# Banded attention and two MoE layers in one program: a shorter routing chain with narrow products, and a new order at both ends of attention

## The reference

```
x   = attention(q, k, v)      # 4 batches, 8 heads, 768 positions, 64 wide
      # own window of |i-j| < 16, and 24 block summaries of 32 keys each
      # (max of keys, mean of values), one softmax over both
y   = moe1(x)                 # 3072 tokens x 512, 8 experts of 512-1024-512
      logits = x @ w_gate
      for (token, expert) by falling logit:    # greedy, one assignment a token
          take it if the token is free and the expert has < 384 tokens
      out[token] = relu(x @ w1[e]) @ w2[e]
out = moe2(y)                 # tokens with y @ w_skip > 0: top-1 expert,
                              # y + gate * ffn(y); others are copied
```

## Time and profile before

| | |
|---|---|
| median of 3 runs | 844.89 us |
| the profiled execution | 845.31 us, span 843.5 us |
| PE matmul busy | 797.3 us (95%) |
| VectorE busy | 465.2 us (55%) |
| ScalarE, GpSimd busy | 228.2 and 216.0 us |
| granted clock, mean | 0.992 |

### The profile page before, as it was taken

How to read it: one execution, slowest core, us unless ns; L and a number is a source line. 1 busy time by engine, 2 the same in 40 slices (tenths; PEclk the granted TensorE clock), 3 DMA queues, 4 the chain that set the end, 5 groups by cost and what they waited for, 6 DMA issues and landing times.

```text
span 843.5 us, 15049 instructions
## 1 busy us (share of the span) xinstructions
PE 797.3 (95%) x4960; PEld 510.3 (61%) x4960; DVE 465.2 (55%) x2146; ACT 228.2 (27%) x681; POOL 216.0 (26%) x313
## 2 busy tenths in 40 slices
PE   5999997797899999999999999999999999999996
PEld 5878785786345445454554545555577686777762
DVE  6989895677777676776767677607049100000000
ACT  5878785421102121121211212121111111110101
POOL 6888973001021020302102021120300321211110
PEclk9999999899999999999999999999999999999999
DMA  9976650436071440706225071446987999898983
GB/s 260 279 235 208 222 151 2 181 129 224 6 262 51 142 170 3 283 26 222 90 75 211 26 261 51 148 164 240 361 321 293 414 372 348 308 338 310 332 318 105
DMA packets 64506, 171.66 MB, mean 204 GB/s; under 512 B 5585, under 2 KB 5585, under 8 KB 64449
## 3 DMA queue, kind: packets, MB, share of 16 engines
q1 hardware_dynamic: 54512, 143.70, 48.3%
q0 software_dynamic: 6480, 20.91, 6.8%
q10 hardware_dynamic: 3456, 6.29, 1.9%
HBM read 148.41 MB, written 22.81 MB: 203 GB/s over the span
## 4 chain that ended last, share of the span: by engine, by line
PE 75%; DVE 14%; DMA 4%; issue 3%; POOL 3%; ACT 1%; DVEq 0%; SPq 0%; POOLq 0%; ACTq 0%
PE bank L1433 16%; PE bank L1447 16%; PE bank L1575 11%; PE bank L1557 11%; DVE junk L987 4%; PE bank L1301 4%; PE bank L1328 3%; PE bank L1310 3%; PE bank L1506 2%; DMA weights<-in_moe_w 1%; PE bank L1298 1%; PE bank L1422 1%; PE bank L1633 1%; PE bank L1601 1%; PE bank L1646 1%
## 5 line engine op out<-in xcount | busy, mean ns | idle before, releaser
L1433 PE MATMUL bank<-features,weights 128*128 128x384 f32 x512 | 182.3, 497 | 0.6 <-ACT features L749 0.6
L1447 PE MATMUL bank<-weights 128*128 128x512 f32 x384 | 179.2, 602 | 0.0
L987 DVE TENSOR_SCALAR_CACHE_REDUCE junk<-Vt,cand 128x192 bf16<-128x192 f32 x376 | 136.1, 410 | 4.8
L1433 PEld LDWEIGHTS bank<-features,weights 128*128 128x128 f32 x512 | 89.5, 191 | 50.6 <-issue 5.6
L1557 PEld LDWEIGHTS bank<-x2T,weights 128*128 128x128 f32 x896 | 102.2, 192 | 5.9 <-issue 5.9
L1557 PE MATMUL bank<-x2T,weights 128*128 128x128 f32 x896 | 102.6, 275 | 0.0
L1447 PEld LDWEIGHTS bank<-weights 128*128 128x128 f32 x384 | 66.8, 190 | 58.5 <-issue 56.5
L1575 PE MATMUL bank<-weights,h2T 128*128 128x512 f32 x224 | 98.8, 593 | 0.4 <-ACT h2T L816 0.4
L1147 DVE SCALAR_TENSOR_TENSOR o<-bank,gate,x 128x512 f32<-128x512 f32 x14 | 10.5, 751 | 154.5 <-PE bank L1575 154.4
L754 ACT ACTIVATE weights<-bank 128x384 f32<-128x384 f32 x64 | 31.4, 490 | 141.4 <-PE bank L1433 141.4
L1575 PEld LDWEIGHTS bank<-weights,h2T 128*128 128x128 f32 x224 | 41.3, 190 | 46.5 <-issue 46.5
(11 more groups left out here) (324 smaller groups left out, 1048.3 us busy)
## 6 DMA issues: line engine op xcount, KB each, us to landing
weights<-in_moe_w SPq DMA_DIRECT2D x52, 2048.0 KB, 9.6
vw<-in_vwin SPq DMA_DIRECT2D x16, 576.0 KB, 4.9
qc<-in_qT SPq DMA_DIRECT2D x16, 384.0 KB, 5.3
kc<-in_kT SPq DMA_DIRECT2D x16, 384.0 KB, 5.8
vc<-in_vT SPq DMA_DIRECT2D x16, 384.0 KB, 7.4
x_rows<-xr SPq DMA_DIRECT2D x24, 256.0 KB, 2.2
y_rows<-weights ACTq DMA_DIRECT2D x24, 256.0 KB
weights<-x_rows,gidx POOLq DMA_INDIRECT x24
```

The lines of the kernel that those rows point to most:

```text
L987: ins = ve.tensor_scalar(junk[:, c, :], Vt[:, :], cand[:, c:c + 1].bitcast(fp32), 0.0, ALU.is_ge, ALU.add, accum_out=cnt[:, c:c + 1])
L1433: ins = mm(HB[r % 2][:, 0:CAP], w1[:, c, 128 * r:128 * r + 128], xgT[:, c, :], start=(c == 0), stop=(c == KC - 1))
L1447: ins = mm(YB[j % 2][:, :], hT[:, r, 128 * j:128 * j + 128], w2[:, r, :], start=(r == 0), stop=(r == FC - 1))
```

## The change

- Narrow products: CNT, TAU, BAS go to 8, 8 and 2 columns; BASN is accumulated into BAS through shifted columns of `rowt`.
- VectorE's chain after the rounds: two operations on oneE are fused into others, the ranks are prepared while PE makes the base, and the expert's number is sent after the row totals, not before; oneE itself is made after the slots. For the first list of tokens, fold and ids are taken some operations earlier.
- End of attention: the first maximum and V are made in two parts, 18 tiles during groups 42 to 45, the last 6 tiles after the last logits. PE transposes six tiles of x before the rounds, and has fillers there.
- Start of attention: SP loads a pair's value windows after the next pair's queries and keys; VectorE takes pair 1's block maxima earlier and its key windows before the first reciprocal; PE has seven products that nothing reads while it waits for the first scores.
- The three gathered columns have a semaphore each; window 1 allows its work one round earlier, 161 units for 145.

```
-        VTP, CNT, TAU = SM[:, 0:256], SM[:, 256:256 + WIDE], SM[:, 384:384 + WIDE]
+        VTP, CNT, TAU = SM[:, 0:256], SM[:, 256:264], SM[:, 384:384 + E]
-            for u in range(NB):
+            load_qk(0)
+            load_columns(0)
+            for u in range(1, NB):
                 load_qk(u)
+                load_v(u - 1)
                 load_columns(u)
-                load_v(u)
+            load_v(NB - 1)
...
+            block_maxima(0)
             first_windows(0, NG)
             block_sums(0)
             maxima(0)
+            block_maxima(1)
             maxima(1)
+            first_windows(1, 1)
             recip(0)
-            first_windows(1, 1)
             maxima(2)
             block_sums(1)
...
+            known, final = slice(0, NT - TB), slice(NT - TB, NT)
...
+                if n == NG * (U - 2):
+                    dve.wait_ge(s["logit_in"], B - 1)
+                    best_of(known)
+                if n == NG * (U - 2) + 1:
+                    dve.wait_ge(s["rev_ready"], 1)
+                    first_of(known)
+                if n == NG * (U - 2) + 2:
+                    others_out(known)
+                if n == NG * (U - 2) + 3:
+                    open_values(known)
             logits_in(B - 1)
             dve.wait_ge(s["logit_in"], B)
+            best_of(final)
+            first_of(final)
+            others_out(final)
+            open_values(final)
...
                 o.step(ve.tensor_reduce(m, src, X, ALU.max))
+                if first_list:
+                    fold_out(ids_of)
                 o.step(ve.tensor_tensor(tmp, src, bc(m, shape, 2), ALU.is_equal))
-                if ids_of is not None:
+                if first_list:
+                    ids_out(ids_of)
+                elif ids_of is not None:
                     fold_out(ids_of)
...
-                o.step(ve.tensor_scalar(oneE[:, :], TAU[:, 0:E], tau[:, :], None, ALU.is_equal))
-                o.step(ve.tensor_tensor(oneE[:, :], oneE[:, :], revE[:, :], ALU.mult))
+                o.step(ve.scalar_tensor_tensor(out=oneE[:, :], in0=TAU, scalar=tau[:, :], in1=revE[:, :],
+                                               op0=ALU.is_equal, op1=ALU.mult))
                 o.step(ve.tensor_reduce(oneM[:, :], oneE[:, :], X, ALU.max))
-                o.step(ve.tensor_scalar(oneE[:, :], oneE[:, :], oneM[:, :], None, ALU.is_equal))
+                o.step(ve.scalar_tensor_tensor(out=t1[:, :, :], in0=bc(oneE[:, :], full, 1), scalar=oneM[:, :], in1=V[:, :, :],
+                                               op0=ALU.is_equal, op1=ALU.mult))
+                o.step(ve.tensor_reduce(mx[:, :], t1[:, :, :], X, ALU.add))
...
+                ve.tensor_copy(rowt[:, 1:3], scn[:, :, NT - 1]).then_inc(s["rows_ready"], 1)
+                o.step(ve.scalar_tensor_tensor(out=rank[:, :, :], in0=scn[:, :, :], scalar=float(-BIG_SLOT), in1=GT[:, :, :],
+                                               op0=ALU.add, op1=ALU.subtract))
                 o.step(ve.tensor_scalar(e_f[:, :], oneM[:, :], -1.0, float(E), ALU.mult, ALU.add))
...
                 ve.tensor_copy(e_i[:, :], e_f[:, :]).then_inc(s["expert_ready"], 1)
+                dve.wait_ge(s["base_mm"], ph + 1)
                 for h in range(2):
+                    o.step(ve.scalar_tensor_tensor(out=rank[:, h, :], in0=rank[:, h, :], scalar=BAS[:, h:h + 1],
                                                    in1=GT[:, h, :], op0=ALU.add, op1=ALU.mult))
...
                 o.step(ve.tensor_scalar(sel[:, :], slot[:, :], CAP - 0.5, None, ALU.is_lt))
+                o.step(ve.tensor_scalar(oneE[:, :], oneE[:, :], oneM[:, :], None, ALU.is_equal))
...
+            pe.wait_ge(s["pads_ready"], 1)
+            for _ in range(7):
+                mm(LG[0:32, 0:128], wg2[:, 0, :], wg2[:, :, :].rearrange("p c e -> p (c e)"), start=True, stop=True)
             pe.wait_ge(s["zeros_ready"], NB)
...
             logit_rows(B - 1)
+            for t in range(4):
+                x_rows_tile(t)
...
-                    return [0] + [0, 0, 6] + [6] * (ROUNDS - 3) + [15, 28, 4, 8]
+                    return [0] + [0, 6] + [9, 6, 6] * 5 + [16, 22, 4, 8]
...
-                if j == 0:
-                    pe.wait_ge(s["xg_in"], 16 * CT * (k + 1))
+                pe.wait_ge(s[f"xg_in{j}"], 16 * (k + 1))
...
+                keep_busy(w, 3)
                 pe.wait_ge(s["v_ready"], w + 1)
...
+                if w == 0:
+                    x_rows_tile(4)
+                    x_rows_tile(5)
+                keep_busy(w, 2)
                 for n in range(ROUNDS):
                     pe.wait_ge(s["cnt_ready"], ROUNDS * w + n + 1)
-                    mm(CNT, same_e[:, :], cnt[:, :].unsqueeze(1).to_broadcast([128, WIDE // 8, 8]),
-                       start=True, stop=True).then_inc(s["cnt_mm"], 1)
+                    mm(CNT, same_e[:, :], cnt[:, :], start=True, stop=True).then_inc(s["cnt_mm"], 1)
...
-                mm(BAS, tri[:, :], rowt[:, :], start=True, stop=True)
-                mm(BASN, ones_bf[:, :], rowt[:, :], start=True, stop=True).then_inc(s["base_mm"], 1)
+                mm(BAS, tri[:, :], rowt[:, 1:3], start=True, stop=False)
+                mm(BAS, ones_bf[:, :], rowt[:, 0:2], start=False, stop=True).then_inc(s["base_mm"], 1)
```

More of the change, by code:

```diff
@@ L106, in banded_attention_two_moe_layers @@
         steps3 = sb("steps3", [128, 3, 3], i32)
-        diag = sb("diag", [E, WIDE])
+        diag = sb("diag", [E, E])
         tau = sb("tau", [128, 1])
@@ L114, in banded_attention_two_moe_layers @@
         scn = sb("scn", [128, 2, NT])
-        rowt = sb("rowt", [128, WIDE], bf16)
-        base = sb("base", [128, 4])
+        rowt = sb("rowt", [128, 3], bf16)
+        rank = sb("rank", [128, 2, NT])
         slot = sb("slot", [128, NT])
@@ L380, in load_weights @@
                 if rows_first:
-                    sp.wait_ge(s["xg_in"], 16 * CT)
+                    for j in range(CT):
+                        sp.wait_ge(s[f"xg_in{j}"], 16)
                 sp.dma_start(W2[:, 2 * par, :].rearrange("p (c f) -> p c f", c=FC),
@@ L608, in _ @@
             keep_ids(0)
-            pool.wait_ge(s["xg_in"], 16 * CT)
+            for j in range(CT):
+                pool.wait_ge(s[f"xg_in{j}"], 16)
             with pool.Fori(1, E) as ph:
@@ L615, in _ @@
                 keep_ids(ph)
-                wait(pool, "xg_in", 16 * CT * (ph + 1))
+                for j in range(CT):
+                    wait(pool, f"xg_in{j}", 16 * (ph + 1))
                 o.leave(E)
@@ L908, in evac_pT, with bc, part_of, best_of @@
                 ve.tensor_copy(pT[:, n % 2, :], PT[n % 2][0:KW, :]).then_inc(s["prob_evac"], 1)
+            def bc(ap, shape, axis):
+                return ap.unsqueeze(axis).to_broadcast(shape)
+            known, final = slice(0, NT - TB), slice(NT - TB, NT)
+            def part_of(ts):
+                return [128, ts.stop - ts.start, E]
+            def best_of(ts):
+                o.step(ve.tensor_reduce(mx[:, ts], LM[:, ts, :], X, ALU.max))
+                o.step(ve.tensor_tensor(t1[:, ts, :], LM[:, ts, :], bc(mx[:, ts], part_of(ts), 2), ALU.is_equal))
+            def first_of(ts):
+                o.step(ve.tensor_tensor(t1[:, ts, :], t1[:, ts, :], bc(revE[:, :], part_of(ts), 1), ALU.mult))
+                o.step(ve.tensor_reduce(first[:, ts], t1[:, ts, :], X, ALU.max))
+            def others_out(ts):
+                o.step(ve.tensor_tensor(t1[:, ts, :], t1[:, ts, :], bc(first[:, ts], part_of(ts), 2), ALU.is_equal))
+                o.step(ve.tensor_scalar(t1[:, ts, :], t1[:, ts, :], -NEG, NEG, ALU.mult, ALU.add))
+            def open_values(ts):
+                o.step(ve.tensor_tensor(V[:, ts, :], LM[:, ts, :], t1[:, ts, :], ALU.add))
             def logits_in(b):
@@ L955, in first_max @@
                 o.step(ve.tensor_tensor(is_first, tmp, bc(first[:, 0:count], shape, 2), ALU.is_equal))
-                if ids_of is not None:
+                if ids_of is not None and not first_list:
                     ids_out(ids_of)
@@ L1010, in search @@
                                                        op0=ALU.logical_shift_left, op1=ALU.bitwise_xor))
-                ve.tensor_scalar(diag[:, 0:E], ident[0:E, 0:E], cand[0:E, 0:1].bitcast(fp32), None, ALU.mult) \
+                ve.tensor_scalar(diag[:, :], ident[0:E, 0:E], cand[0:E, 0:1].bitcast(fp32), None, ALU.mult) \
                     .then_inc(s["tau_diag"], 1)
                 dve.wait_ge(s["tau_mm"], ph + 1)
-                o.step(ve.tensor_reduce(tau[:, :], TAU[:, 0:E], X, ALU.max))
-                o.step(ve.tensor_scalar(oneE[:, :], TAU[:, 0:E], tau[:, :], None, ALU.is_equal))
-                o.step(ve.tensor_tensor(oneE[:, :], oneE[:, :], revE[:, :], ALU.mult))
+                o.step(ve.tensor_reduce(tau[:, :], TAU, X, ALU.max))
+                o.step(ve.scalar_tensor_tensor(out=oneE[:, :], in0=TAU, scalar=tau[:, :], in1=revE[:, :],
```

(4 more changed lines are left out.)

49 lines of the change are left out of this document (23 added, 26 removed).

## The result

The changed kernel takes **854.5 us** (median of 4 runs, 852.81 to 856.17) against 845.15 us for the kernel before beside it (844.82 to 845.77): ratio 1.0096, 95% interval 1.0068 to 1.0124, so it is slower by 1%. (The ratios here are the ones on record with their intervals; they differ by up to 0.0016 from the quotient of the two medians.) Forecast were 831.4 us and a range of 827 to 837, and faster. The profiled execution took 852.81 us with a span of 851.0.

The account below looks back on a forecast made before the run. PE work was taken as the main bound (75% of the span, VectorE 14%). V(2) earlier -5.3, lead -3.45, windows 2 to 7 -4.8: -13.5 from 845.31 gave 831.8, adjusted to the median 831.4 us; range 827 to 837.

Parts of the forecast that it names:

- the lead: Window 1: PE does 161 units for 145, so four second-layer products no longer follow, -3.45 us.
- rival D: Six full windows: PE, being ahead, waits for late gathered columns, up to 3.54 us each; 853 us, chance 0.04.
- The expert's number: After tau: number and weight load come 1.8 us later; weights landed long before use in window 0, so no charge.
- Narrow products in the full windows: Windows 2 to 7: each 8-column count product saves 0.03 us of PE's chain, 3.1 us in all.
- Rival B: Full windows: narrow products cost what wide ones did, next weights uncovered; 3.1 + 1.0 go, 835.5 us, chance 0.09.
- Windows 2 to 7 as a sum: PE-bound windows: count products 3.1, tau and base 1.0, shorter VectorE chain 0.7; -4.8 us, bounds 1 and 7.
- Start: Start of attention: keys loaded earlier and PE at full clock bring the fourth scores forward, -1.8 us, bounds 0.8 and 2.6.
- the signs: Start of attention: fourth scores near 12.8, first scores in about 1.05 us, V's first transpose near 147.5.
- Window 0: First window: head -0.9, rounds -1.0 and the search's tail -0.8 us.
- The store of tile 1: Head of window 0: if it again takes 4.58 us to land, round 1 goes only at 154.5, no gain.
- the forecast 191: Tail of window 0: sign that gidx, for the first list of tokens, would be done near 191.
- rival A: The ends give little: interleaved transfers, late store, gather and fillers taking 1.5 in window 1; 834.8 us, chance 0.18.

Follow-up runs that it names:

- e1_early: The changed kernel with the expert's number sent early again, as before the change, lead of 16 units kept: 848.19 us, ratio 1.002.
- e3_both: The changed kernel with the expert's number early and the old window 1 list (145 units, no lead): 837.84 us, ratio 0.9891.
- e7_lead17: The changed kernel with the expert's number early and one more unit in window 1's list (162 for 161): 840.01 us, ratio 0.9928.
- e8: The changed kernel with the number early, the old window 1 list and another split of windows 3 to 7's 209 units over the rounds: 839.15 us.
- e11: The kernel of e3_both with the old start of attention put back: 838.19 us, ratio 0.9897.
- e12: The kernel of e3_both with the first row transposes waiting for all three gathered columns: 839.08 us, ratio 0.9924.
- e13_late17: The changed kernel, expert's number late, with one more unit in window 1's list (162 for 161): 852.39 us, ratio 1.0078.
- e9_before_lead: The kernel before the change with only the new window 1 list (161 units for 145): 872.55 us, ratio 1.0303.
- e2_oldroom: The changed kernel with the old window 1 list (145 units, no lead), expert's number late: 840.92 us, ratio 0.9925.
- e10_both_again: The kernel of e3_both, unchanged, run again on another chip: 840.52 us, ratio 0.9936.
- e4_before_late: The kernel before the change with only the expert's number moved late: 845.39 us, ratio 0.9991.
- e5_before_narrow: The kernel before the change with only the small products' width cut from 128 to 8 columns: 843.06 us, ratio 0.9962.

## Why the prediction was wrong, step by step

**The step that failed is the lead, -3.45.** I wrote that four products "no longer follow" and that "this is where the idle 3.7 us of 206-228 go". Three things are wrong in it.
1. *Window 1 had little room.* With the number early, V(1) to V(2) takes 49.1 with the lead of 16 (e1_early) for 46.9 without (e3_both): +2.2. With 17, where the list completes 162 units for 142 without the lead, it takes 51.2 (e7_lead17). Some 0.9 of that is a clock fall, which e8, e11 and e12 show without the lead (47.7 to 47.9): some +3.4, and from V(7) on 340.8 remain for 344.6: -3.8. The idle time of the earlier trace rows is some 0.3 us in each round, too little for another product of 0.68; a round of 9 units takes 2.04 and its count product where it took 1.86. So the lead of 17 gave back what it had cost and hardly more.
2. *The phase.* I took the windows behind as unchanged because they get the same 209 units. They get whole items, and 16 units shift which ones fall together: e1_early less e7_lead17 is 1.6 us in each of windows 4 and 5, and 8.1 us from V(2) to the end. Nothing in my text had this mechanism.
3. *The rows.* Being ahead, TensorE meets the gathers. This was rival D, with a price of up to 3.54 a window; I gave it 0.04. It happened: 9.0 us of waits in after, 12.6 in e13_late17, 15.4 in e9_before_lead. In after that is 1.3 on average in each of seven waits, below the 2.25 from which I had let it decide; with the short rounds and a clock fall it was enough. My reason against it, evenly spread columns, put the first one near 351; in window 4 of after it landed at 354.94, for what comes next.

**The expert's number, "so nothing is charged".** I had only asked when the weights are used, not what their load stands in front of. Leaving 2.3 us nearer to V, the second load is in the way of the gathers: it lands 6.9 us behind V(4) in after, 2.7 behind it in e3_both, and the gathers' landing medians are 6.1 us with the number late (after, e2_oldroom) for 4.0 to 4.3 with it early (e3_both, e1_early). Price: 854.5 to 848.2 us with the lead of 16, 852.4 to 840.0 with 17; without a lead 840.9 to 837.8, where the intervals overlap, and e10_both_again's 840.5 leaves nothing of it. It is an interaction; neither e4_before_late nor e2_oldroom shows it alone.

**Narrow products in the full windows, 3.1.** Rival B had the mechanism right. The rows that I held against the rule of the Trainium skill, TensorE: Matmul & The Clock Gate (LDWEIGHTS), that a weight load hides behind the running product, measured the product and not the one behind it. After shows 2.04 + 0.01 for 1.99 + 0.06. By that rule a product of 8 columns covers almost nothing of the next load, and the trace agrees. Of the 3.1 + 1.0 that B takes away some 2 were there all the same, 0.35 a window in e5_before_narrow, at the places where VectorE waits.

**Windows 2 to 7 as a sum, -4.8.** About right without the lead: V(2) to V(7) takes 249.1 in e3_both for 252.9, -3.8 in five windows. 0.35 a window come with the narrow width (e5_before_narrow). The rest, some 0.4 a window, I put down to the shorter chain; no run has that by itself.

**Start, -1.8.** In the one profile of after the fourth scores began at 12.81 for the earlier trace rows's 14.95, the first scores took 1.36 us for 1.90 (I had named 1.05), and V(0) came 2.0 earlier: the signs were there, and the timed runs don't show the gain. e11_old_start, without all of it, is no slower.

**Window 0, -2.7 from V(0) to V(1).** 46.3 for 48.1: -1.8. Rounds of 1.855 for 1.91 as forecast. The store of tile 1 landed in 3.98 us, so round 1 was held about as I had feared. gidx came at 191.45, near the forecast 191. TensorE then stood idle for 0.96 and 1.47 us, and the granted clock of 194-198 was 0.68: the 12 fillers behind the first count took 2.91 us, where e3_both at full clock has 1.58, and the first product came at 202.69 instead of 200.35. My sum had none of that, rival A had 1.5 for it.

**The sum.** From after to e3_both the profiled span falls by 15.4: window 0 0.1, window 1 3.3, window 2 1.0, window 3 5.1, windows 4 to 6 6.8, from V(7) on 0.6, less 1.5 for a later V(0). Of a forecast of -13.5 some 5 to 9 were there without the lead and with the number early (the ratios 0.9936 of e10_both_again and 0.9891 of e3_both; from V(0) 7.4 and 7.5 less than before in the profiles), and the lead with the late number turned them into a loss.

**The better kernel.** The kernel of e3_both and that of e11_old_start both beat the two kernels: 0.9891 and, run again, 0.9936 of the time before for the first, 0.9897 (0.9883 to 0.9912) for the second.

## What to carry to other kernels

Where work is dealt out in whole items between the steps of another engine's chain, shifting the list by a few units changes every later round: count the items out, round by round, against the chain's period, ahead of costing a lead as pure gain. Work done ahead is a gain only in a round with a whole item's idle time, and it brings the engine sooner to the next transfer. A load that leaves later is to be charged not only against its own use, but against every transfer that it will then share the engines with.

## What the runs showed of the hardware

- Three indirect gathers that leave 0.3 to 0.5 us ahead of V(4) land in a median of 6.1 us where a 2,048 KB weight load of the same core is under way until 6.9 us behind V(4) (after; 6.1 in e2_oldroom too), and in 4.0 us where it lands 2.7 behind it (e3_both).
- An 8-column product ahead of a full-width one saves nothing on TensorE: 2.04 + 0.01 for 1.99 + 0.06. Where VectorE waits for the product it saves 0.05 us, 0.18 for 0.23 (e5_before_narrow).
- Behind the head of window 1 the granted clock fell in six executions with the new chain (after, e7, e8, e11, e12, e13; 0.68 on average in 194-198 us of after) and not in four (e1, e2, e3, e10). TensorE's idles ahead of it were the same with and without: 0.96 and 1.47 us in after, 0.96 and 1.48 in e8 and in e3_both, which kept 1.00. Without the lead the fall costs about 1 us: window 1 takes 47.7 to 47.9 with it (e8, e11, e12), 46.5 to 46.9 without (e2, e3, e10). What decides it isn't shown; V(0) doesn't, for it fell with V(0) at 147.3 (after) and at 151.8 (e11) and not at 148.8 (e3).
- A wait of 2.3 us for a gather in window 3 of after was followed by a granted clock of 0.57 in 301-305 us.
- A 384 KB load in the crowded start took 7.46 us when issued at 2.65 (after) and 15.96 to 18.03 us when issued at 8.62 to 10.76 (seven executions of the new start).
